# When the second-half weights of a routed expert layer are loaded, and where TensorE reads the tile table

## The reference, cut to what matters

```python
attn = windowed attention plus block summaries over q, k, v     # (2, 8, 768, 64)
x = attn, transposed to rows                                    # (1536, 512)
x = sum over 4 experts of p[:, e] * (relu(x @ w1[e]) @ w2[e])   # dense: every row, every expert
# routed layer, 8 experts, one expert for a row:
do_compute = x @ w_skip > 0
e_idx = argmax(x @ w_gate); gate_w = its softmax probability
out = x
out[rows of expert e] += gate_w * (relu(x @ w1[e]) @ w2[e])     # w1 (8, 512, 1024), w2 (8, 1024, 512)
```

## Time and profile before

| what | value |
|---|---|
| median of 3 runs | 755.8 us (753.83, 755.80, 758.25) |
| the profiled execution | 753.83 us, its span 752.1 us |
| granted TensorE clock, mean over the span | 0.989 |
| PE busy | 726.7 us, 97% of the span |
| DVE, ACT, POOL busy | 297.6, 209.2, 68.0 us (40%, 28%, 9%) |
| bytes by DMA | 79.44 MB, mean 106 GB/s |

### The profile page before, as it was taken

The page is one execution under the profiler, slowest core; times in us unless marked ns, Lnnn a source line. Parts: engine busy times, 40 slices in busy tenths (PEclk is TensorE's granted clock), DMA queues, the critical chain, the costliest instruction groups (busy, mean ns, idle before and its releaser), DMA issues.

```text
span 752.1 us, 12583 instructions
## 1 busy us (share of the span) xinstructions
PE 726.7 (97%) x4612; PEld 604.1 (80%) x4613; DVE 297.6 (40%) x874; ACT 209.2 (28%) x504; POOL 68.0 (9%) x97
## 2 busy tenths in 40 slices
PE   4699999999999999999999999999999999999997
PEld 3488898888998989899898989989898986454454
DVE  4978674452433212143321214331524254544341
ACT  3745454451321102032210203222020211543330
POOL 2531000000000000000000000000101002432321
PEclk9789999999999999999999999999999999999999
DMA  9794622212222000022200001252020259599900
GB/s 205 188 223 96 145 64 61 47 31 91 97 78 72 1 1 0 0 61 84 79 0 0 0 0 52 88 196 85 1 85 1 85 207 373 195 401 393 396 24 22
DMA packets 78613, 79.44 MB, mean 106 GB/s; under 512 B 54216, under 2 KB 54492, under 8 KB 78176
## 3 DMA queue, kind: packets, MB, share of 16 engines
q1 hardware_dynamic: 75904, 74.11, 31.3%
q0 software_dynamic: 2656, 4.66, 1.9%
HBM read 71.02 MB, written 8.24 MB: 105 GB/s over the span
## 4 chain that ended last, share of the span: by engine, by line
PE 87%; DMA 5%; DVE 4%; issue 1%; POOL 1%; SPq 1%; ACT 1%; POOLq 0%; DVEq 0%
PE ps L1373 23%; PE ps L1375 23%; PE ps L1374 23%; PE ps L1669 4%; PE ps L1641 4%; DMA sets<-in_moe_w 3%; PE ps L1435 2%; PE ps L1407 2%; PE ps L1559 1%; PE ps L1421 1%; PE ps L1386 1%; DMA acc<-stage 1%; PE ps L1548 1%; PE ps L1654 1%; PE ps L1396 1%
## 5 line engine op out<-in xcount | busy, mean ns | idle before, releaser
L1373 PE MATMUL ps<-xt_hi,w_hi 128*128 128x384 f32 (+1 forms) x508 | 173.0, 340 | 0.0
L1375 PE MATMUL ps<-xt_hi,w_lo 128*128 128x384 f32 (+1 forms) x508 | 170.2, 335 | 0.0
L1374 PE MATMUL ps<-xt_lo,w_hi 128*128 128x384 f32 (+1 forms) x508 | 170.0, 335 | 0.0
L752 ACT ACTIVATE h_hi<-ps 128x384 fp32r<-128x384 f32 x128 | 62.9, 492 | 361.7 <-PE ps L1375 361.6
L1373 PE MATMUL ps<-w_hi,h_hi 128*128 128x512 f32 x384 | 151.9, 396 | 0.0
L1375 PE MATMUL ps<-w_hi,h_lo 128*128 128x512 f32 x384 | 150.0, 391 | 0.0
L1374 PE MATMUL ps<-w_lo,h_hi 128*128 128x512 f32 x384 | 149.8, 390 | 0.0
L985 DVE SCALAR_TENSOR_TENSOR h_lo<-ps,h_hi 128x384 fp32r<-128x384 f32 x128 | 71.1, 556 | 161.8 <-ACT h_hi L752 161.7
L1373 PEld LDWEIGHTS ps<-xt_hi,w_hi 128*128 128x128 f32 x508 | 95.4, 188 | 1.7 <-issue 0.8
L1374 PEld LDWEIGHTS ps<-xt_lo,w_hi 128*128 128x128 f32 x508 | 95.5, 188 | 0.5
L1375 PEld LDWEIGHTS ps<-xt_hi,w_lo 128*128 128x128 f32 x508 | 95.3, 188 | 0.0
(11 more groups left out here) (196 smaller groups left out, 601.2 us busy)
## 6 DMA issues: line engine op xcount, KB each, us to landing
sets<-in_moe_w SPq DMA_DIRECT2D x72, 512.0 KB, 7.8
stage<-in_moe_w SPq DMA_DIRECT2D x24, 512.0 KB, 3.8
stage<-in_k SPq DMA_DIRECT2D x16, 192.0 KB, 4.1
acc<-in_v SPq DMA_DIRECT2D x4, 768.0 KB, 6.4
x_rows<-acc SPq DMA_DIRECT2D x4, 768.0 KB, 4.1
out_rows<-acc SPq DMA_DIRECT2D x4, 768.0 KB, 5.7
acc<-in_moe_w POOLq DMA_DIRECT2D x4, 512.0 KB, 4.7
acc<-in_moe_w SPq DMA_DIRECT2D x4, 512.0 KB, 4.5
```

What stands on the lines that cost most here:

```text
L752: nc.scalar.activation(h_hi[:, f, :], ps[:, f % 2, 0:GT], ACT.Relu).then_inc(h_hi_ok, 1)
L1373: mm(dst, a_hi, b_hi, start=start, stop=False)
L1374: mm(dst, a_hi, b_lo, start=False, stop=False)
L1375: return mm(dst, a_lo, b_hi, start=False, stop=stop)
```

## The change

SyncE: set 3's first layer is issued as two pieces ahead of the list and two behind the gather of tile 3, where three were ahead of the list and one directly behind it. VectorE: the two register loads for tile 3 stand ahead of the wait for the list. TensorE: the wait for the table and its register loads stand behind layer 2, `turn_h` and `first_rows` of tiles 2 and 3, and `turn_h(3)` comes ahead of `first_rows(3)`.

```diff
             load_set(2, 1, range(2, PIECES))
-            load_set(3, 0, range(3))
+            load_set(3, 0, range(2))
             for e in (1, 2):
...
-            load_set(3, 0, range(3, PIECES))
             sp.wait_ge(list_in, 16 * SIDES)
             sp.wait_ge(gathered[STARS + 1], 16)
+            load_set(3, 0, range(2, PIECES))
             load_set(3, 1)
...
             columns = [column_at(i) for i in range(3, SLOTS)]
+            third, at_third = set_at(3), waits_at(3)
             dve.wait_ge(list_in, 16 * SIDES)
             for i in range(3, SLOTS):
                 make_ids(i, columns[i - 3])
-            third, at_third = set_at(3), waits_at(3)
...
             layer1(3, 1)
+            for _ in layer2_steps(3, 0, bank_x(1)):
+                pass
+            turn_h(3)
+            first_rows(3)
             pe.wait_ge(table_ok, 1)
             tiles = pe.value_load(table[0:1, 0:1], min_val=1, max_val=TILES)
-            third = set_at(3)
-            for _ in layer2_steps(3, 0, bank_x(1)):
-                pass
-            first_rows(3)
-            turn_h(3)
-            layer1(4, third)
+            layer1(4, set_at(3))
```

## The result

Over 20 runs of each kernel, measured side by side, the changed kernel takes 758.51 us (756.37 to 760.68) and the one before 754.68 us (752.70 to 758.25): 3.8 us more, a ratio of 1.0051 with a 95% interval of 1.0040 to 1.0061. The change makes the kernel slower by half a per cent, just at the bound that was set for "no change". The median of before over 20 runs is 1.1 us under that of the three runs shown ahead of the prediction. The profiled execution took 757.18 us with a span of 755.5 us, 3.4 us more than before's.

What follows compares the result with a forecast made beforehand. The prediction took the weight stream's landing of set 5.0 as the bound, TensorE only 0.29 us behind. Terms 2.7 + 0.7 + 0 + 0 = 3.4 us on the 755.8 us median gave 759.2 us, range 755.5 to 762.8.

Steps and rivals of the forecast that it cites:

- The bound: Routed layer, at 678.22 us: the weight stream's landing of set 5.0 decides, later than TensorE by only 0.29 us.
- Two pieces: Weight stream behind the gather: two more 512 KB pieces make set 5.0 land 2.7 us later (2.4 to 3.0).
- Row numbers: VectorE after the list: two further register loads delay the first row number, and so the gather, by 0.7 us (0 to 0.7).
- Gather and list without a piece beside them: List read and tile 3's gather: gather might gain 0 to 0.5 us, list's gain is lost in VectorE's loads; 0 taken.
- TensorE's table wait and the order of turn_h: TensorE ahead of tile 3: layer 1 comes between 0.7 us earlier and 0.6 us later; 0 taken.
- over 3 us in hand: TensorE from tile 3 to tile 6: slack of over 3 us, so a shift at tile 3 does not matter.
- Sum: Set 5.0 lands 2.7 + 0.7 + 0 + 0 = 3.4 us later, all passed to TensorE: 759.2 us on the median.
- Rival A: Behind the new pause ahead of tile 6 the clock falls, costing 1.7 to 3.3 us more: 760.9 to 762.5 us; chance 0.27.
- A pause of 3 to 4 us ahead of tile 6: Sign: TensorE pauses 3 to 4 us before layer 1 of tile 6; prediction wrong if under 2 us.
- set 5.0 landing after 679: Sign in the weight stream: set 5.0 lands near 680.7 us; prediction wrong if before 679.
- B: Set 5.0 no longer late, TensorE alone sets the end: 754.8 us, half-way form 756.8; chance 0.15 for both.
- C: Set 3.0 too late for tile 4: TensorE stops at 661.57 already, pause split in two, 760 to 761 us; chance 0.04.

Runs made afterwards that it cites:

- sp_only: Kernel before with SyncE's edit alone (two pieces of set 3's first layer behind the gather): 757.65 us against 754.29, ratio 1.0047.
- pe_only: Kernel before with TensorE's edit alone (turn_h before first_rows for tile 3, register loads behind both): 754.90 us against 754.29, ratio 1.0006.
- sp_beside: Kernel before with set 3's first layer split two pieces ahead of the list, two directly behind it: 754.18 us against 754.55, ratio 0.9996.
- sp_four: Kernel before with all four pieces of set 3's first layer behind the gather: 758.72 us, ratio 1.0051.
- dve_only: Kernel before with VectorE's edit alone (two register loads ahead of the wait for the list): 754.76 us against 754.29, ratio 1.0006.
- after_filled: Changed kernel with 12 filler matmuls in front of layer 1 of tile 6: 756.99 us against 754.55 for the kernel before, ratio 1.0036.

## Why the prediction was right, step by step

- **The bound** (set 5.0's landing, TensorE 0.3 us behind it): right. Moving pieces out of the stream and into it moves T, and with 14 pieces TensorE has no wait for a set.
- **Two pieces, 2.7 us with the ends 2.4 and 3.0:** measured 2.6 to 3.3 (29.0 to 29.4 against 26.1 to 26.4). The five profiles with 18 pieces and the five with 16 are 2.8 us apart on average, so the term was right to 0.1 us; between the two kernels' first profiles it was 3.0.
- **Row numbers, 0.7 us:** 0.8 us in all three profiles of the changed kernel (4.08, 4.07, 4.08 against 3.28 us behind the list's issue). The list's read takes longer in some executions: without VectorE's edit the first row number comes 3.2 to 3.5 us behind its issue (before, sp_only, pe_only, sp_beside, sp_four), so the cost is 0.5 to 0.9 us, 0.7 on average. By time alone it is not resolved (dve_only 1.0006).
- **Gather and list without a piece beside them, 0 taken:** the gather took 2.6 us (issue at 648.93, SyncE's wait over at 651.55) where it was 2.61; over the runs it is 2.49 to 2.69 us without a piece and 2.57 to 2.65 with one. The rule of the Trainium skill (DMA: Bandwidth & Descriptors, Latency and other measured facts) that a lighter load makes the fixed cost smaller is seen at most as 0.1 us between one piece and none; the 0.5 us worked out from it did not come. With two and three pieces beside it the gather did take longer, 3.10 and 3.42 us; how much of that is the fixed cost no run tells.
- **TensorE's table wait and the order of turn_h, 0:** right in the time (pe_only 1.0006), not in the bound given with it, at most 0.6 us later for layer 1 of tile 3. Counted from the list's issue it was 2.2 and 1.5 us later in the first and third profile of the changed kernel. The "over 3 us in hand" took that up.
- **Sum, 3.4 us:** span + 3.4, set 5.0 + 3.4, in the profiled execution; 3.8 over 20 runs (3.0 to 4.6). That both numbers come so close is partly luck. In the profiled execution the shift was 3.8 us (0.8 + 3.0), and the stages ahead happened to end 0.4 us sooner. The median of 758.51 us is near the forecast 759.2 because the median of before was taken 1.1 us too high and the shift 0.4 us too low. What holds without luck is the average over profiles: T - L is 37.7 to 37.9 us in the four of the changed kernel, the filled one included, and 34.0, 34.5 and 34.8 in before, pe_only and sp_beside, 3.4 us apart.
- **Rival A:** the clock did fall, behind 3.13 and 2.94 us of pause ahead of tile 6 in two profiles (sp_only and the second of the changed kernel, 1.3 and 1.6 us on span - T, under the 1.7 to 3.3 us that were worked out from the attention stage), not behind 2.56 us in the third of the changed kernel. It was counted as a rival to the forecast, with 0.27; it is a part of it that is in some executions and not in others. Its share in the 3.8 us is not settled: 3.4 us without it lie inside the interval of 3.0 to 4.6. The clock falling behind a pause is as the Trainium skill has it (TensorE: Matmul & The Clock Gate, Part 1).
- **"A pause of 3 to 4 us ahead of tile 6":** wrong in the profiled execution (0.54 us), by something that the prediction did not have: TensorE late ahead of tile 3. By the prediction's own sign ("wrong if TensorE's pause there is under 2 us") it would have failed there; the sign was badly chosen, since a pause tells when TensorE arrives as well as when the weights do. The other sign, set 5.0 landing after 679, held (680.69), and in the second and third profile and in sp_only the pause is 2.94, 2.56 and 3.13 us. TensorE's lateness only used up slack and changed nothing in the sum.
- **Rivals B and C:** B did not happen, for the reason given (two pieces more to make good). C did not either; even with four pieces behind the gather tile 4's layer 1 ran without a wait. The split of the pause that C speaks of did come, at tile 5 instead of tile 4: 1.17 us there in the second profile of the changed kernel, 2.94 us in sp_four.

## What to carry to other kernels

A transfer that is moved from idle time on the DMA engines into a saturated stretch costs its whole transfer time (here 1.3 to 1.7 us for 512 KB), if the end of that stretch releases the bounding engine, even when nothing seems to wait for the transfer itself; look for the idle time that it leaves. Work moved into a wait is free only up to what the wait has left: here three register loads already filled all but 0.4 us of it. And a longer wait of TensorE can cost more than its length, because the clock may fall behind it; whether the loss counts depends on whether another wait stands behind it.

## What the runs showed of the hardware that was not expected

TensorE's results can come later than its matmul rows say. In the first and third profile of the changed kernel the transposes at 651.46 and 651.95 (650.75 and 651.24) look done by 652.3 (651.6), but ScalarE and VectorE, which wait for them, start at 653.96 and 654.65 (653.20 and 653.24), with "remote" as releaser.

```profile
653.96 0.60 ACT L829 ACTIVATE acc<-ps 128x512 f32<-128x512 f32 x1 [3.35 <-remote]
```
```profile
654.65 0.42 DVE L1234 COPY acc<-ps 128x256 f32<-128x256 f32 x1 [2.54 <-remote]
```

In both, TensorE's two register loads stand right behind these transposes; but they do so too in the second profile, in pe_only and in after_filled, where nothing was late. The cause is open. Also, the clock fell behind pauses of 2.88, 2.94 (twice) and 3.13 us and not behind 2.56, 2.18, 1.97 and 1.84 us. Ahead of the first pause of each of these profiles the granted clock had been 1.00 since 629 us.
